# Attention and two gated products on one core: weights split once and kept in DRAM as pairs

## The reference

```python
scores = np.matmul(q, k.transpose(0, 1, 3, 2)) / np.sqrt(64)
scores = cap * np.tanh(scores / cap)
attn = np.exp(scores - np.max(scores, axis=-1, keepdims=True))
attn = attn / (np.sum(attn, axis=-1, keepdims=True) + 1e-09)
x = np.matmul(attn, v)            # to 1792 tokens x 768
x = (1 / (1 + np.exp(-(x @ w_gate)))) * (x @ w_val) @ w_out      # 768 -> 1536 -> 768
h = x @ w_in                                                     # 768 -> 2048
y = (h * np.cos(h)) @ w_out2                                     # 2048 -> 768
```

## Time and profile before

| | |
|---|---|
| time, median of 3 runs | 1376.86 us (1375.03 to 1378.82) |
| span of the profiled execution, first to last instruction | 1378.3 us |
| PE busy | 1291.2 us, 94% |
| POOL busy | 963.9 us, 70% |
| DVE busy | 847.8 us, 62% |
| ACT busy | 574.7 us, 42% |
| moved by DMA | 140.65 MB, 102 GB/s |

### The profile page before, as it was taken

How to read it: one execution, slowest core, us unless ns; L and a number is a source line. 1 busy time by engine, 2 the same in 40 slices (tenths; PEclk the granted TensorE clock), 3 DMA queues, 4 the chain that set the end, 5 groups by cost and what they waited for, 6 DMA issues and landing times.

```text
span 1378.3 us, 22562 instructions
## 1 busy us (share of the span) xinstructions
PE 1291.2 (94%) x6468; PEld 1146.6 (83%) x6468; DVE 847.8 (62%) x1249; ACT 574.7 (42%) x1085; POOL 963.9 (70%) x778
## 2 busy tenths in 40 slices
PE   7889998899889999889989999989997999999999
PEld 5558987789778898778968899878897899999988
DVE  7992347868876335777887523677788743313840
ACT  6772135546543114555654311555555431102620
POOL 4436797668775678666876478876787757777883
PEclk9999999999999999999999999999999999999999
DMA  3223343224322334313432233422253223333341
GB/s 91 83 73 94 128 142 93 72 69 152 113 92 83 99 119 142 98 56 91 153 117 75 78 106 130 142 83 68 91 157 109 68 89 114 104 109 108 121 129 42
DMA packets 69693, 140.65 MB, mean 102 GB/s; under 512 B 27664, under 2 KB 30736, under 8 KB 69648
## 3 DMA queue, kind: packets, MB, share of 16 engines
q1 hardware_dynamic: 66048, 134.50, 31.6%
q10 hardware_dynamic: 3600, 5.51, 1.1%
HBM read 134.48 MB, written 5.51 MB: 102 GB/s over the span
## 4 chain that ended last, share of the span: by engine, by line
PE 60%; DVE 20%; issue 11%; ACT 8%; DVEq 1%; DMA 0%; ACTq 0%; POOL 0%; POOLq 0%
PE acc L387 16%; PE acc L388 16%; PE acc L389 16%; DVE tmp_b L770 4%; PE t_ps L326 4%; DVE prob L674 3%; DVE tmp_b L767 3%; PE s_ps L317 2%; PE s_ps L318 2%; DVE h_lo L779 2%; DVE rowmax L662 2%; ACT prob L514 2%; PE acc L335 2%; ACT tmp_b L601 2%; ACT prob L507 2%
## 5 line engine op out<-in xcount | busy, mean ns | idle before, releaser
L240 POOL TENSOR_TENSOR w_lo<-w_raw,w_hi 128x768 fp32r<-128x768 f32 (+1 forms) x256 | 506.9, 1980 | 21.4
L237 POOL TENSOR_SCALAR w_hi<-w_raw 128x768 fp32r<-128x768 f32 (+1 forms) x256 | 250.3, 978 | 220.4 <-PE acc L389 186.2
L387 PE MATMUL acc<-h_hi,w_hi 128*128 128x448 f32 x672 | 259.4, 386 | 0.9 <-DVE h_lo L779 0.9
L389 PE MATMUL acc<-h_hi,w_lo 128*128 128x448 f32 x672 | 249.6, 371 | 0.0
L388 PE MATMUL acc<-h_lo,w_hi 128*128 128x448 f32 x672 | 249.6, 371 | 0.0
L387 PE MATMUL acc<-x_hi,w_hi 128*128 128x448 f32 x576 | 211.3, 367 | 2.1 <-issue 2.1
L388 PE MATMUL acc<-x_lo,w_hi 128*128 128x448 f32 x576 | 211.1, 366 | 0.0
L389 PE MATMUL acc<-x_hi,w_lo 128*128 128x448 f32 x576 | 211.0, 366 | 0.0
L745 DVE TENSOR_TENSOR tmp_b<-acc,tmp_a 128x448 f32<-128x448 f32 x48 | 30.0, 624 | 194.0 <-PE acc L389 194.0
L514 ACT ACTIVATE prob<-prob,shift,cap_abs 112x448 f32<-112x448 f32 x192 | 144.2, 753 | 11.1 <-DVE shift L664 10.6
L662 DVE TENSOR_REDUCE rowmax<-prob 112x2 f32<-112x896 f32 x96 | 103.7, 1080 | 67.1 <-ACT prob L507 66.3
(11 more groups left out here) (77 smaller groups left out, 2109.7 us busy)
## 6 DMA issues: line engine op xcount, KB each, us to landing
w_raw<-w SPq DMA_DIRECT2D x208, 384.0 KB, 3.0
w_raw<-w SPq DMA_DIRECT2D x48, 512.0 KB, 3.5
qk_raw<-qk SPq DMA_DIRECT2D x48, 448.0 KB, 3.5
v_raw<-v SPq DMA_DIRECT2D x48, 112.0 KB, 2.7
yT<-y_sb ACTq DMA_DIRECT2D x24, 224.0 KB, 2.0
cap_in<-cap ACTq DMA_DIRECT2D x1, 0.5 KB, 3.1
```

Of the source, the lines that this page charges most:

```text
L237: return e.tensor_scalar(out, in_, 1.0, 1.0, ALU.mult, ALU.mult)
L240: return e.tensor_tensor(out, whole, f32(hi), ALU.subtract)
L387: e.matmul(out[:, 0:S], w_hi[p][:, wb, :], a_hi[:, kb, :], start=first, stop=False)
L389: return e.matmul(out[:, 0:S], w_lo[p][:, wb, :], a_hi[:, kb, :], start=False, stop=last)
```

## The change

In batch 0 the weights are loaded and split as before. Behind it, SP stores each half of `w_hi` and `w_lo` into a DRAM tensor (`kept`, named w1_pair to w4_pair): four stores for each unit. POOL may overwrite `w_hi[p]` and `w_lo[p]` only when the stores from there have landed (`s_wkept`). In batches 1 to 3, SP loads the high and the low part of each half straight into `w_hi` and `w_lo`, four transfers for each unit, each half as soon as PE is done with that half two units back (`s_acc`), and PE waits for these loads (`s_wpair`) in place of POOL's split. POOL splits no weights there, only q, k and v. Before the first load of batch 1 SP waits for all stores. The second half of a unit always begins at block `HALF_MAX` of the buffer. All loops are written out on all engines, so that addresses and counts are constants. The order of the operations on PE, DVE and ACT stays.

```diff
@@ program
-        with e.Fori(0, B - 1) as b:
+        for b in range(B):
             for stage in (1, 2, 3, 4):
-                product(stage, b, True)
-        for stage in (1, 2, 3, 4):
-            product(stage, B - 1, False)
+                product(stage, b, b < B - 1)
...
@@ pairs
+        for j in range(n):
+            body(j, j % 2, j // 2, bool(peel) and j >= n - 2)
...
@@ SP
+                def load_pair(j, p, u):
+                    for h in range(2):
+                        part = slice(h * HALF_MAX, h * HALF_MAX + blk)
+                        e.wait_ge(s_acc, 2 * (u - 2) + h + 1 + 2 * CREDIT)
+                        for c, half_of in enumerate((w_hi, w_lo)):
+                            e.dma_start(f32(half_of[p])[:, part, :],
+                                        kept[stage][bass.ds(j, 1), h, c, :, :, :].rearrange("a p k m -> (a p) k m")).then_inc(s_wpair[p][h], 16)
...
+                    if is_first(b):
+                        load_raw(j, p, u)
+                        if u > 0:
+                            keep(u - 1)
+                    else:
+                        load_pair(j, p, u)
...
+                if b == 1 and stage == 1:
+                    for p in range(2):
+                        e.wait_ge(s_wkept[p], 16 * 2 * UNITS)
...
+            def keep(u):
...
+                for h in range(2):
+                    part = slice(h * HALF_MAX, h * HALF_MAX + blk)
+                    e.wait_ge(s_wsplit, 2 * u + h + 1 + 2 * CREDIT)
+                    for c, half_of in enumerate((w_hi, w_lo)):
+                        e.dma_start(kept[stage][j, h, c, :, :, :], f32(half_of[p])[:, part, :]).then_inc(s_wkept[p], 16)
...
@@ POOL
+                    if is_first(b):
+                        e.wait_ge(s_acc, 2 * (u - 1) + 2 * CREDIT)
+                        if u >= 2:
+                            e.wait_ge(s_wkept[p], 64 * uses)
...
@@ PE
-                            e.wait_ge(s_wsplit, 2 * u + h + 1 + 2 * CREDIT)
+                            if is_first(b):
+                                e.wait_ge(s_wsplit, 2 * u + h + 1 + 2 * CREDIT)
+                            else:
+                                e.wait_ge(s_wpair[p][h], 32 * pair_uses(stage, b, i))
```

More of the change, by code:

```diff
@@ L107, in build @@
     s_whi, s_wsplit, s_held = sem("w_hi_done"), sem("w_split"), sem("gpsimd_waits_held")
+    s_wpair = [[sem(f"w_pair_loaded{p}{h}") for h in range(2)] for p in range(2)]
+    s_wkept = [sem(f"w_pair_kept{p}") for p in range(2)]
     s_qkld = [sem(f"qk_loaded{p}") for p in range(2)]
@@ L122, in build @@
     s_out = [sem(f"y_stored{p}") for p in range(2)]
+    kept = {stage: nc.dram_tensor(f"w{stage}_pair", (u, 2, 2, P, blk, P), F32, kind="Internal").ap()
+            for stage, u, blk in ((1, U1, BLK1), (2, U2, BLK2), (3, U3, BLK3), (4, U4, BLK4))}
     def f32(tile):
@@ L131, in program, with is_first, pair_uses @@
         heads_alone()
-        with e.Fori(0, B - 1) as b:
+        for b in range(B):
             for stage in (1, 2, 3, 4):
-                product(stage, b, True)
-        for stage in (1, 2, 3, 4):
-            product(stage, B - 1, False)
-    def pairs(e, n, body, peel=False, peel_first=False):
[L141 to L153, removed]
+                product(stage, b, b < B - 1)
+    def is_first(b):
+        return b == 0
+    def pair_uses(stage, b, i):
+        return (b - 1) * (UNITS // 2) + units_of[stage][1] // 2 + i + 1
+    def pairs(e, n, body, peel=False, peel_first=False):
+        for j in range(n):
+            body(j, j % 2, j // 2, bool(peel) and j >= n - 2)
+    blocks_of = {1: BLK1, 2: BLK2, 3: BLK3, 4: BLK4}
     units_of = {1: (U1, 0), 2: (U2, OFF2), 3: (U3, OFF3), 4: (U4, OFF4)}
@@ L217, in unit @@
                         load_v(*front)
+                if b == 1 and stage == 1:
+                    for p in range(2):
+                        e.wait_ge(s_wkept[p], 16 * 2 * UNITS)
                 pairs(e, n, unit, is_peeled(stage, beside))
+                if is_first(b) and stage == 4:
+                    keep(UNITS - 1)
+            def keep(u):
+                stage = next(s for s in (1, 2, 3, 4) if u < units_of[s][1] + units_of[s][0])
+                j, blk, p = u - units_of[stage][1], blocks_of[stage], u % 2
+                for h in range(2):
+                    part = slice(h * HALF_MAX, h * HALF_MAX + blk)
+                    e.wait_ge(s_wsplit, 2 * u + h + 1 + 2 * CREDIT)
+                    for c, half_of in enumerate((w_hi, w_lo)):
+                        e.dma_start(kept[stage][j, h, c, :, :, :], f32(half_of[p])[:, part, :]).then_inc(s_wkept[p], 16)
             program(e, heads_alone, product)
@@ L281, in unit @@
                     u = b * UNITS + off + j
[L282 to L289, removed]
+                    uses = off // 2 + i
+                    if is_first(b):
+                        e.wait_ge(s_acc, 2 * (u - 1) + 2 * CREDIT)
+                        if u >= 2:
+                            e.wait_ge(s_wkept[p], 64 * uses)
+                        for h in range(2):
+                            part = slice(h * HALF_MAX, h * HALF_MAX + blk)
+                            e.wait_ge(s_wld[p][h], 16 * (uses + 1))
+                            rounded(w_hi[p][:, part, :], w_raw[p][h][:, 0:blk, :]).then_inc(s_whi, 1)
+                            e.wait_ge(s_whi, 2 * u + h + 1)
+                            rest(w_lo[p][:, part, :], w_raw[p][h][:, 0:blk, :], w_hi[p][:, part, :]).then_inc(s_wsplit, 1)
                     if front:
-                        e.wait_ge(s_wsplit, 2 * u + 2 + 2 * CREDIT)
+                        if is_first(b):
+                            e.wait_ge(s_wsplit, 2 * u + 2 + 2 * CREDIT)
                         split_v(*front)
```

21 lines of the change are left out of this document (13 added, 8 removed).

## The result

| | before | after |
|---|---|---|
| time, median | 1375.94 us (4 runs, 1374.08 to 1378.82) | 1308.72 us (4 runs, 1307.07 to 1308.97) |
| ratio | | 0.948 (95% interval 0.944 to 0.953) |
| span of the profiled execution | 1378.3 us | 1306.9 us |
| forecast | | 1331 us (1315 to 1357) |

The direction and the place were right, the size was not: 67 us were gained where 46 were forecast. Three lines of the page of after: its span, the busy time of each engine, and the load and store queue of SP (packets, MB, share of 16 engines).

A forecast was written before the change was run, and what follows sets the result against it. PE was taken to wait for DVE, which stands still while POOL works on weights. 1378.3 - 29.2 - 5.7 - 12.3 + 1 = 1332.1 us of span, so 1331 us, range 1315 to 1357.

The forecast's parts named there:

- The rival that it does nothing: DVE's long instructions have another cause than POOL's weight split, so PE's waits stay: 1377 us, within 5; chance 0.03.
- Removing the split: Batches 1 to 3 without POOL's weight split: PE's waits in batches 1 and 2 shrink, 29.2, 5.7 and 12.3 us off.
- the 16 waits: PE's waits for `pt_lo` and `prob` in batches 1 and 2, 30.8 us: 0.1 us left for each, 29.2 off.
- the start of stage 4: Two PE waits in batches 1 and 2, 8.1 us: 1.2 us left of each, 5.7 off; ends 8.1 and 3.2.
- the clock: Batches 1 and 2: time given away by PE's lowered clock, 13.8 us; 1.5 left, 12.3 off; ends 0 and 13.8.
- The first rival: Stages 2 and 4, batches 1 and 2: `pt_hi` or POOL's rest keeps PE waiting; 1345 to 1357 us, chance 0.13.
- The loops: Writing out loop turns and register work on all engines: put at 0, with ends of -3 and +3 us.
- The pace: Matmul pace in steady parts of batch 0 and early batch 1: left as is; ends -4 and +10 us.
- Pair loads: Batches 1 to 3, stages 1 and 3: 1.57 MB a unit, 215 GB/s, nothing on the path; cover about 3 us.
- Stores in batch 0: Stages 1 and 3: 0.79 MB in and 1.57 MB out a unit, 318 GB/s; cost 1 us, ends 0 and 10.
- The rival of the transfers as the bound: Stages 1 and 3 of batch 0: slow stores give 10.4 us a unit, 52 us more, 1383 us; chance 0.07.
- a time below 1315: Whole kernel: every wait gone, a fast pace and something gained from the loops; chance 0.04.

The follow-up runs named there:

- the idle split: The changed kernel, with POOL in batches 1 to 3 still doing as much splitting, but on buffers nobody uses: 1367.34 us, 0.988 of before.
- loops alone: The kernel before with all its loops written out on all engines, nothing else changed, POOL still splitting in every batch: 1362.98 us, 0.985 of before.
- the second trace of before: The unchanged kernel before, run and profiled once more: 1377.3 us in one run, 1375.4 us of span.
- pieces issued back to back: The changed kernel with POOL's weight split in batch 0 cut into pieces of two blocks (256 columns) everywhere: 1296.47 us, 0.939 of before.
- the kernel with pieces beside attention only: The changed kernel with batch 0's split in two-block pieces only where attention is worked on, whole instructions elsewhere: 1294.31 us, 0.934 of before.

## Why the prediction fell short

**What bounds the kernel: right.** DVE held up by POOL's weight instructions was the cause, as the run with the idle split shows. The rival that it does nothing is out.

**Removing the split: the mechanism right, the size too small by about 9 us.** From loops alone to after, batches 1 and 2 fell from 669.4 to 613.4 us, by 56.0; the sum had 29.2 + 5.7 + 12.3 = 47.2. I had left 1.6 us for the 16 waits, 2.4 us for the start of stage 4 and 1.5 us of the clock, 5.5 in all. After shows none of them in these batches: not one wait, and a clock of 1.00 in every stage. The margins of 0.2 to 0.4 us in ACT's `pt_hi` were enough in every unit. POOL's earlier split of q and k, for which I kept 1.2 us at each start of stage 4, cost nothing there. Two waits of 1.0 us for `z_lo` at the start of stage 3, which I had seen and left out of the sum, went as well. The first rival (the next in line is late) did not come about at all.

**The loops: the step that failed.** The largest term that the sum lacked is the loops. I put 0, with ends of -3 and +3, because stage 1 of batch 3 has six turns of the small loop and no idle time. That row was the wrong one to read. Batch 3 stands outside the loop over batches and has nothing beside it. Where the turn goes far, from stage 4 back to stage 1, PE stood 0.9 to 1.4 us each time, and stage 4, with attention beside it, was 3 us longer in each batch with the loops. Measured: 13 us against the second trace of before, 16 against the first, and 21 by the ratio of 0.985. This term alone would have put the time at 1310 to 1318 us, around the low end of the range. It does not stand by itself: beside the pairs most of the loops cost 4 to 9 us, and the pairs gained 58 us with these loops in place. Both terms were too small.

**The pace: named, with the right size.** The 4 us of the three slow stages were gone in after. They were gone in the second trace of before too, and that trace was no shorter in its four batches, so the change did not take them away.

**Pair loads: right.** Leaving them out changed nothing. No load was waited for.

**Stores in batch 0: the share was right, and the 1 us was not needed.** Stage 1 of batch 0 moved 309 GB/s at a share of 0.85, which as an estimate would be 364 at 1.00, nearer the burst (390) that I took than the 309 of the earlier trace rows. The loads were issued 7.8 us before POOL took them up (7.9 worked out), and the first half was ready 4.1 us ahead of PE (4.5 worked out, 4.2 before). With 335.0 us, batch 0 was no longer than without stores (337.1). The rival of the transfers as the bound did not come about. The transfers overlap: stage 1 of batch 0 issued 23 loads and 46 stores, at medians of 5.2, 2.8 and 3.3 us from issue to landing, which one behind the other would be 260 us in a stage of 94.9. So the fixed 2.0 us for each transfer that the Trainium skill (DMA: Bandwidth & Descriptors, Anatomy of one DMA) gives did not add up; the page has it from transfers issued by GpSimd, and here SP issues them.

In the sum: 1332.1 - 1306.9 = 25.2 us, of which 15.9 are loops and slow stages, 5.5 are residues that vanished, 2.0 are the waits for `z_lo`, 1 the stores, and 0.8 are left. That it closes so well is partly luck. These are single traces; 6.9 of the 15.9 lie in the heads alone, which scatter by 6 us within one kind of kernel, and in the trace of after that stretch is only 3.1 us shorter than in the first trace of before. Against the medians the forecast was off by 22 us. The prediction had given 0.04 to a time below 1315, "with every wait gone, a fast pace and something gained from the loops". That is what came.

Open: why the longest waits for `pt_lo` are longer with loops (3.0 against 2.3 us) while their total is the same, what the rest of the 3 us in each stage 4 is, and what sets the pace of 206 or 203 ns. No run was made on any of these alone.

## What to carry to other kernels

An engine that is idle a third of the time, and that no wait beside the weight products names, can still set the time, by holding up another one: look for instructions whose maximum is far above their minimum, and see what the neighbour engine was doing at that moment. If its work can't go, make its instructions shorter, as long as it keeps up. And cost a loop where it turns far or where its engines wait, not in a stretch that has no turn of the outer loop and nothing to wait for.

## What the runs showed of the hardware

- POOL's instructions on SBUF, with one input or two, held up DVE's `tensor_scalar` of 448 columns for less than their own length: 0.88 us at the most beside copies of 1.05 us, 2.13 us beside subtractions of 2.4 (the idle split, 2570 - 440 ns). Each of the 118 slowed instructions ended 0.24 to 0.26 us behind the end of one POOL instruction, and none was held through two. With pieces issued back to back, 3 of 25 were.
- Not every DVE instruction is held up. In batches 1 and 2 of the kernel before, those that were have all their operands in SBUF: `tensor_scalar` (`prob`, 441 to 2566 ns) and those with two SBUF inputs (L770, 624 to 2246 ns; `h_lo`, 609 to 2119). Those with an operand in PSUM never were, nor was the row maximum (`tensor_reduce`, 1068 to 1087 ns). So `pt_lo` was late because it stood behind `prob`, and never slow itself:

```profile
L678 DVE TENSOR_TENSOR pt_lo<-t_ps,pt_hi x96: 606/611/626, 549.8 to 1121.7; 112x448 fp32r<-112x448 f32 x96
```

- Short pieces on POOL are dearer: a subtraction takes 0.74 us for 256 columns and 1.86 for 768, so three pieces cost 3 x 0.74 - 1.86 = 0.36 us more than one instruction.
- With loads and stores mixed the DMA engines moved 326 GB/s at a share of 0.90 in stage 3 of batch 0 of the kernel with pieces beside attention only, and PE was never idle:

```profile
277.20:337.10 59.90, 59.90 (x302) 55.45 (x300) 49.67 (x59) 35.17 (x62) 50.43 (x35) 1.00 0.90 326
```

- A steady row of matmuls of 448 columns ran at 203 or at 206 ns each for a whole stage at a clock of 0.99 to 1.00, in the same kernel: stage 1 of batch 1 at 206 in the first trace of before and 203 in the second.
